# Attention, MLP and routed experts: token rows reordered in 32x32 blocks by VectorE instead of turned by TensorE

## The chip, the cores and the metric

The kernel runs on one core of a Trainium2 chip. The metric is the device time of one execution in microseconds (us), the median of three runs of the kernel before: 533.54 us (533.23 to 533.99). Two numbers stand beside it for the execution that was profiled: its time was 533.14 us, and its span, which is the stretch that the trace covers, was 531.4 us.

## The reference, cut to what matters

Three stages follow each other. All inputs are float32.

```python
# 1 attention with decay, B=2, H=8, S=768, D=64, in blocks of 64 positions -> x [1536, 512]
# 2 gated MLP, d_model 512, d_ff 1536
g = x @ w_gate
x2 = (g * sigmoid(g) * (x @ w_val)) @ w_out
# 3 top-1 experts: E=8, F=1024
logits = x2 @ router
e = argmax(logits, axis=1)
gate = softmax(logits)[e]
out[token] = gate * (relu(x2[token] @ w1[e]) @ w2[e])
```

So stage 3 needs each token's row of x2 (512 numbers) and its 8 logits, gathered by expert.

## The kernel before

There is no scheduler. Each engine has its program written out in order, and semaphores tie them together. SP (SyncE) issues nearly all loads in one queue, so an instruction on SP that waits holds back everything behind it. POOL (GpSimd) issues the gathers and scatters.

Each float32 product is made of three reduced products: a tile is split into a high part (a copy to fp32r by ScalarE, ACT) and a low part (a subtraction by VectorE, DVE), and TensorE (PE) multiplies high by high, high by low, and low by high. `split_expert` does this for one of the 8 pieces of an expert's weights, `tokens` for an expert's rows.

**MLP.** The 1536 tokens are three groups of 512. The result of a group, `x2f`, has the features on the partitions and the tokens along the free axis. An expert needs rows that can be gathered, so the tokens must come to the partitions. `rows(fin, t, where)` in the PE program turns one tile of 128 tokens with four 128x128 transposes (L974), and `rows_out` copies it from PSUM to `x2`, beside the 8 logits. `store_rows` stores 128 rows of 520 numbers to `x2_rows` in DRAM. Groups 0 and 1 are turned between other products: group 0 behind `held_out` j = 2, 4, 6, 8 and group 1 behind the hidden units f = 1 to 4 of the last group. Group 2 is turned in the tail of the MLP.

**Experts.** An expert has two tiles of 120 rows (`ROWS`), so 240 places. Tiles 0 and 1 of expert 0 have paths of their own (`gather_a`, `gather_b`, `transpose_a`, `transpose_b`). For experts 1 to 7, POOL gathers the rows into `gx[0]` and `gx[1]`, and `transpose_rows(x)` in the PE program turns them back with two times four transposes (L1163), for expert 1 ahead of the last part of expert 0, and for the others inside the expert before, after `outward(x, par, 3)`. ACT and DVE split the turned rows from PSUM into `exh` and `exl`.

In expert x the PE order is `hidden(0)`, `hidden(1)`, `outward(0)`, `hidden(2)`, `outward(1)` and so on: `hidden(f)` is 12 matmuls of 240 columns (L1174), `outward(f)` 6 matmuls of 512 (L1184). `outward(f)` waits for `ehl`, the low part of relu, which DVE makes after ACT has made `ehh`. In the same steps ACT and DVE split piece f of the next expert's weights, and at f = 5 the next expert's rows (`tokens`). SP loads the weights of an expert in four loads of 1 MB (`load_expert`), each as soon as DVE has split the piece pair that lay in that slot. In `last_expert` tile 0 goes with the hidden steps, and all of tile 1 follows (`outward_tile`, L1217).

Empty places hold an index (2048) that the gather skips.

Of the kernel before, what the change touches and what calls it, by code (L numbers as in the profile page):

```python
# [38 lines left out]
ROWS_BEHIND = (2, 4, 6, 8)  # L39
# [21 lines left out]
EMPTY = 2048  # L61
# [37 lines left out]
def bass_linear_attention_mlp_moe(nc, attn_in, lam_rows, mlp_w, router_w, expert_w, out):  # L99
    ctx = ExitStack()  # L100
    with ctx:
# [7 lines left out]
        x2_rows = nc.dram_tensor("x2_rows", [N, ROW], F32, kind="Internal").ap()  # L109
# [100 lines left out]
        x2 = sb("x2", [P, GTT, ROW], F32, region2)  # L210
# [22 lines left out]
        ys = [sb(f"ys{i}", [P, DM], F32, region2) for i in range(2)]  # L233
        region2.close()
# [73 lines left out]
        x2_stored = [sem(f"x2_stored{i}") for i in range(GTT)]  # L308
        logits_psum = sem("logits_psum")
# [23 lines left out]
        gx_landed = [sem(f"gx_landed{i}") for i in range(2)]  # L333
        exh_ready = sem("exh_ready")
# [19 lines left out]
        def expert_bufs(par):  # L354
            return ((ewh0, ewl0), (ewh1, ewl1))[par]

# [102 lines left out]
        def _(sp):  # L459
# [10 lines left out]
            for n in range(4, NT):  # L470
                sp.wait_ge(scores_ready, n - 3)
                if n >= 6:
                    sp.wait_ge(qs_ready, n - 5)
                keys_and_queries_in(n % 4, n)
                sp.wait_ge(o_ready, n - 3)
                rows_in(n % 4, n)
                if n == 6:
                    for h in range(2):
                        sp.dma_start(flat(h), mlp_w[0][:, h * GT:(h + 1) * GT]).then_inc(first_halves[h], 16)
# [69 lines left out]

            sp.wait_ge(mwl_ready, splits(1, NF1 - 1))  # L550
# [4 lines left out]
            sp.wait_ge(route, (NG - 1) * STEPS + 3)  # L555
            for t in range(GTT):
                sp.wait_ge(rows_ready, (NG - 1) * GTT + t + 1)
                sp.dma_start(x2_rows[(NG - 1) * GT + t * P:(NG - 1) * GT + (t + 1) * P, :],
                             x2[:, t, :]).then_inc(x2_stored[t], 16)
# [3 lines left out]
            n = read_passes(sp)  # L563
            with sp.Fori(2, E) as e:
                load_expert(e, e)

            def later_pass(p):
                with sp.Fori(0, E) as e:
                    load_expert(p * E + e, e)

# [6 lines left out]
        def _(pool):  # L577
# [78 lines left out]
            last_early_row = pool.to_reg((NG - 1) * GT - 1)  # L656

# [5 lines left out]

            def gather_a():
# [3 lines left out]
                for t in range(GTT):  # L668
                    pool.wait_ge(x2_stored[t], 16 * (NG - 1))
                pool.wait_ge(gx_zero, 1)  # L670
# [12 lines left out]
            def gather_b():  # L683
# [3 lines left out]
                for t in range(GTT):  # L687
                    pool.wait_ge(x2_stored[t], 16 * NG)
                pool.wait_ge(idx_ready, 1)
                fetch(gx[1], x2_rows, idx[:, E:E + 1], gx_landed[1])  # L690

            def gather(x):
                pool.wait_ge(gx_read, x * 2)
                pool.wait_ge(expo_ready, x)
                pool.wait_ge(idx_ready, 1)
                for i in range(2):
                    fetch(gx[i], x2_rows, idx[:, x + i * E:x + i * E + 1], gx_landed[i])
# [12 lines left out]
            def first_pass():  # L710
                gather_b()
                pool.wait_ge(gx_read, 1)
                fetch(gx[0], x2_rows, idx[:, 1:2], gx_landed[0])
                pool.wait_ge(expo_ready, 1)
                fetch(gx[1], x2_rows, idx[:, E + 1:E + 2], gx_landed[1])
# [8 lines left out]
            def gather_by_copy(x, base, par):  # L724
# [6 lines left out]
                for i in range(2):  # L731
                    fetch(gx[i], x2_rows, idx_now[:, 2 * par + i:2 * par + i + 1], gx_landed[i])
# [47 lines left out]
        def _(pe):  # L780
# [190 lines left out]
            def rows(fin, t, where):  # L971

                for k in range(KD):
                    last = nc.tensor.transpose(bank[:, where, k * P:(k + 1) * P], x2f[:, k, t * P:(t + 1) * P],  # L974
# [15 lines left out]
            def first_half(g, fin=None):  # L990

                for f in range(HALF):
# [3 lines left out]
                    if fin is not None:  # L996
                        if f == 0:
                            logit_product(fin)
                        if f == 1:
                            pe.wait_ge(route, fin * STEPS + 1)  # L1000
# [1223 lines left out]
```

## Time and profile before

| | |
|---|---|
| median of three runs | 533.54 us |
| the profiled execution | 533.14 us, span 531.4 us |
| PE busy | 522.7 us (98%) |
| DVE busy | 348.7 us (66%) |
| ACT busy | 253.8 us (48%) |
| POOL busy | 73.2 us (14%) |
| the chain that ended last | PE 95%, DMA 1%, issue 1% |
| mean granted TensorE clock | 0.997 of full speed |

The attention stage takes about the first 46 us of the span, the MLP runs to about 335 us, and the experts fill the rest. The chain of waits is almost all PE, so what counts is what PE executes and what makes it wait; other engines count where PE comes to wait for them.

### The profile page before, as it was taken

The numbers are of one execution on the slowest core, as the hardware profiler recorded it, in microseconds if no ns is written. First come the engines' busy times: TensorE is split into PE (matmuls) and PEld (weight loads), VectorE is DVE, ScalarE is ACT, GpSimd is POOL, SyncE is SP. The second block draws the span as 40 slices with busy tenths as digits, with TensorE's granted clock in tenths as the row PEclk, the third lists the DMA queues.
The fourth block names the chain that finished last, engine by engine and source line by source line (L and its number), as shares of the span: only waits on it lengthen the run. The fifth ranks groups of instructions, "written<-read, shape, count | busy, mean of one in ns | idle before, by whom it ended". The sixth has DMA issues, their size and how long they took to land.

```text
span 531.4 us, 8643 instructions
## 1 busy us (share of the span) xinstructions
PE 522.7 (98%) x3279; PEld 443.3 (83%) x3279; DVE 348.7 (66%) x601; ACT 253.8 (48%) x447; POOL 73.2 (14%) x86
## 2 busy tenths in 40 slices
PE   8999999999999999999999999999999999999995
PEld 7998888888888887887888888778888989888893
DVE  7889998787784737644556666567666666766620
ACT  4663564535454325543334534466555455555511
POOL 5761000000000000010000020033022130321101
PEclk9999999999999999999999999999999999999998
DMA  8995224313030305655344566267675665654001
GB/s 282 395 317 199 70 91 158 120 39 140 20 133 7 120 9 183 188 167 208 92 128 152 185 198 237 81 204 256 210 276 195 219 224 205 224 215 153 3 26 37
DMA packets 22570, 84.58 MB, mean 159 GB/s; under 512 B 3836, under 2 KB 3836, under 8 KB 18944
## 3 DMA queue, kind: packets, MB, share of 16 engines
q1 hardware_dynamic: 17664, 71.35, 38.9%
q0 software_dynamic: 3712, 10.54, 6.0%
q10 hardware_dynamic: 1152, 2.13, 1.0%
q8 instruction: 26, 0.43, 0.3%
q14 instruction: 16, 0.13, 0.1%
HBM read 75.32 MB, written 10.27 MB: 161 GB/s over the span
## 4 chain that ended last, share of the span: by engine, by line
PE 95%; DMA 1%; issue 1%; POOL 0%; SPq 0%; POOLq 0%; ACT 0%; DVE 0%
PE bank L947 18%; PE bank L872 16%; PE bank L1174 14%; PE bank L1184 13%; PE bank L880 12%; PE bank L904 6%; PE bank L1088 2%; PE bank L1107 2%; PE bank L830 2%; PE bank L792 2%; PE bank L803 2%; DMA stages<-attn_in 1%; PE bank L1163 1%; PE bank L974 1%; PE bank L1217 1%
## 5 line engine op out<-in xcount | busy, mean ns | idle before, releaser
L1639 DVE TENSOR_TENSOR ewl<-stages,ewh 128x1024 fp32r<-128x1024 f32 x50 | 60.7, 1222 | 17.2 <-ACT ewh L1261 17.2
L1261 ACT ACTIVATE ewh<-stages 128x1024 fp32r<-128x1024 f32 x50 | 52.1, 1052 | 0.3 <-DMA stages<-expert_w 0.3
L1584 ACT ACTIVATE ehh<-bank 128x240 fp32r<-128x240 f32 x48 | 17.8, 370 | 57.8 <-PE bank L1174 51.2
L644 POOL DMA_DIRECT2D stages<-expert_w x8 | 4.6, 577 | 260.4 <-DVE more_hl L1639 185.1
L1184 PE MATMUL bank<-ewh,ehl 128*120 128x512 f32 x96 | 38.0, 396 | 0.0
L1184 PE MATMUL bank<-ewl,ehh 128*120 128x512 f32 x96 | 37.8, 394 | 0.0
L1184 PE MATMUL bank<-ewh,ehh 128*120 128x512 f32 x96 | 37.8, 394 | 0.0
L659 POOL DMA_INDIRECT gx<-x_rows,idx x15 | 22.2, 1481 | 105.3 <-issue 85.1
L1174 PEld LDWEIGHTS bank<-exh,ewh 128*128 128x128 f32 x224 | 32.7, 189 | 4.2
L2132 DVE SCALAR_TENSOR_TENSOR ehl<-bank,ehh 128x240 fp32r<-128x240 f32 x48 | 19.4, 404 | 23.8 <-ACT ehh L1584 23.8
L1174 PE MATMUL bank<-exh,ewh 128*128 128x240 f32 x224 | 34.8, 278 | 0.0
L1174 PE MATMUL bank<-exh,ewl 128*128 128x240 f32 x224 | 34.5, 276 | 0.0
L872 PE MATMUL bank<-xh,gvh 128*128 128x512 f32 x128 | 34.4, 391 | 0.0
L1174 PE MATMUL bank<-exl,ewh 128*128 128x240 f32 x224 | 34.4, 276 | 0.0
L872 PE MATMUL bank<-xl,gvh 128*128 128x512 f32 x128 | 34.2, 389 | 0.0
L872 PE MATMUL bank<-xh,gvl 128*128 128x512 f32 x128 | 34.2, 389 | 0.0
L1174 PEld LDWEIGHTS bank<-exl,ewh 128*128 128x128 f32 x224 | 29.7, 191 | 0.0
L1174 PEld LDWEIGHTS bank<-exh,ewl 128*128 128x128 f32 x224 | 29.6, 190 | 0.0
L1261 ACT ACTIVATE c<-bank 128x512 f32<-128x512 f32 x30 | 17.9, 596 | 24.3 <-PE bank L947 24.3
L880 PE MATMUL bank<-hh,woh 128*128 128x512 f32 x72 | 28.7, 398 | 0.0
L872 PEld LDWEIGHTS bank<-xl,gvh 128*128 128x128 f32 x128 | 24.0, 188 | 5.0
L872 PEld LDWEIGHTS bank<-xh,gvl 128*128 128x128 f32 x128 | 24.0, 188 | 5.0
(292 smaller groups left out, 1240.6 us busy)
## 6 DMA issues: line engine op xcount, KB each, us to landing
stages<-expert_w SPq DMA_DIRECT2D x21, 1024.0 KB, 5.0
stages<-mlp_w SPq DMA_DIRECT2D x23, 768.0 KB, 4.5
stages<-attn_in SPq DMA_DIRECT2D x18, 512.0 KB, 6.9
stage<-expert_w SPq DMA_DIRECT2D x7, 1024.0 KB
stages<-expert_w POOLq DMA_DIRECT2D x8, 512.0 KB, 5.7
stages<-mlp_w SPq DMA_DIRECT2D x13, 256.0 KB, 3.0
stage<-attn_in SPq DMA_DIRECT2D x6, 512.0 KB, 6.7
held<-c SPq DMA_DIRECT2D x12, 256.0 KB, 2.0
```

The source lines that it names most:

```text
L659: nc.gpsimd.indirect_dma_start(out=dst[0:ROWS, :], out_offset=None, in_=src, in_offset=bass.IndirectOffsetOnAxis(ap=at[0:ROWS, :], axis=0) ...
L792: last = mm(bank[:, S_BANK[n % 2] + z, a * CH:(a + 1) * CH], kt[z * D:(z + 1) * D, a, :], qt[z * D:(z + 1) * D, a, :], start=True, stop=True)
L872: last = mm(bank[:, where, :], wt[:, k, :], (xh, xl)[x][:, k, g * GT:(g + 1) * GT], start=(at == 0), stop=(at == 3 * KD - 1))
L880: last = mm(bank[:, d, :], (woh, wol)[w][wo][:, d * P:(d + 1) * P], (hh, hl)[x][h][:, :], start=(f == 0 and n == 0), stop=True, skip_group ...
L904: last = mm(bank[:, d, :], (woh, wol)[w][j % 3 + 1][:, d * P:(d + 1) * P], (hh, hl)[x][j % 3 + 1][:, :], start=(j == 0 and n == 0), stop=True,
L947: last = mm(where, mix(i, w)[:, n * KH * P + k * P:n * KH * P + (k + 1) * P], moving[i][x][:, k, :], start=(first and at == 0), stop=(at = ...
L1174: last = mm(bank[:, H_BANK + f % 2, 0:CAP], expert_bufs(par)[w][:, f, k * P:(k + 1) * P], (exh, exl)[z][par][:, k, 0:CAP], start=(at == 0) ...
L1184: last = mm(bank[0:ROWS, Y_BANK + t, 0:DM], (ehh, ehl)[z][f % 2][:, t * ROWS:(t + 1) * ROWS], expert_bufs(par)[w][:, f, KD * P:], start=(f ...
L1261: return nc.scalar.activation(dst, src, ACT.Copy)
L1584: nc.scalar.activation(ehh[f % 2][:, :], bank[:, H_BANK + f % 2, 0:CAP], ACT.Relu).then_inc(ehh_ready, 1)
L1639: V.tensor_tensor(dst, src, high.bitcast(F32), ALU.subtract).then_inc(inc, 1)
L2132: V.scalar_tensor_tensor(out=ehl[f % 2][:, :], in0=bank[:, H_BANK + f % 2, 0:CAP], scalar=0.0, in1=ehh[f % 2][:, :].bitcast(F32), op0=ALU.max,
```

## The change

Two kinds of turning leave PE.

1. **Groups 0 and 1 of the MLP.** DVE turns a tile with one instruction, a stream transpose, which transposes each 32x32 block of a 128x512 tile on its own and moves no block to other partitions. So a row of `x2` on partition (b, i), with b the block of 32 partitions, holds for each of 16 blocks of 32 tokens a piece of 128 numbers. The blocks are brought to their rows by the store: one store for each b, of 512 pieces of 512 bytes (`store_blocks`). The features of a row lie in another order (`block_order`: k inside, four by four). Group 2 is still turned by PE, and ACT's copy puts it in that order. The logits have a tile (`x2_logits`) and a store of their own, of 32-byte pieces.
2. **Rows of experts 1 to 7.** POOL gathers into `gy`. SP stores both tiles to a DRAM buffer `xg`, waits for that store, and loads `gt` with four loads of 32 partitions, 256 pieces of 512 bytes each, and the logits (`lg`) with a fifth. DVE then makes the turned tiles with one stream transpose each, from `gt` to the same two PSUM banks. SP does the store and the loads of expert e right behind the four weight loads of e.

Also: the tiles `exh` and `exl` are read in two strips of 120 columns with a pitch of 128; ACT and DVE split 128 columns per tile instead of 120; empty places hold the index 1536, a spare row that is gathered like any other; in `last_expert` the first product of tile 1 stands ahead of the wait for the last `ehl`; and the two loads of the first MLP weights (`sig`, `hid`) are issued at attention tile 11 instead of 6, and read by ACT after tile 8 instead of 7.

```diff
 # SP
-                if n == 6:
+                if n == NT - 1:
                     for h in range(2):
                         sp.dma_start(flat(h), mlp_w[0][:, h * GT:(h + 1) * GT]).then_inc(first_halves[h], 16)
...
+            def store_rows(x):
+                for i in range(2):
+                    sp.wait_ge(gy_landed[i], x * 16)
+                    sp.dma_start(xg[i * P:i * P + ROWS, :], gy[i][0:ROWS, :]).then_inc(xg_stored, 16)
+
+            def load_rows(x):
+                sp.wait_ge(xg_stored, x * 32)
+                for b in range(NB):
+                    sp.dma_start(gt[b * BLOCK:(b + 1) * BLOCK, :, :],
+                                 xg[:, b * P:(b + 1) * P].rearrange("(q i) c -> i q c", i=BLOCK)
+                                 ).then_inc(gt_landed, 16)
+                sp.dma_start(lg[:, :, :], xg[:, DM:].rearrange("(t r) e -> r t e", r=P)).then_inc(lg_landed, 16)
...
+            store_rows(1)
+            load_rows(1)
             with sp.Fori(2, E) as e:
                 load_expert(e, e)
+                turn_rows(e)
 # POOL
             def gather(x):
-                pool.wait_ge(gx_read, x * 2)
-                pool.wait_ge(expo_ready, x)
+                if x >= 2:
+                    pool.wait_ge(gt_landed, (x - 1) * (16 * NB))
+                    pool.wait_ge(lg_landed, (x - 1) * 16)
 # PE
-                        if 1 <= f <= GTT:
-                            pe.wait_ge(rows_ready, fin * GTT + f - 1)
-                            rows(fin, f - 1, ROWS_BANK)
...
-                    if f == 4 and more:
-                        transpose_rows(x + 1)
...
-                transpose_rows(1, True)
...
+                outward_tile(x, 0, 1)
                 pe.wait_ge(ehl_ready, x * NF2 + NF2)
                 outward_tile(x, NF2 - 1, 0)
-                for f in range(NF2):
+                for f in range(1, NF2):
                     outward_tile(x, f, 1)
 # ACT
+            def store_blocks(fin, b):
+                act.wait_ge(rows_ready, fin * GTT + GTT)
+                act.dma_start(x2_rows[fin * GT:(fin + 1) * GT, b * P:(b + 1) * P].rearrange("(q i) c -> i q c", i=BLOCK),
+                              x2[b * BLOCK:(b + 1) * BLOCK, :].rearrange("i (q c) -> i q c", c=P)
+                              ).then_inc(x2_stored[b], 16)
 # DVE
+            def turn_rows(fin, t):
...
+                V.transpose(x2[:, t * DM:(t + 1) * DM].rearrange("p (a j k) -> p a k j", a=NB, k=KD),
+                            x2f[:, :, t * P:(t + 1) * P].rearrange("p k (a i) -> p a k i", a=NB)).then_inc(rows_ready, 1)
...
+            def turn_tokens(x, i):
+                dve.wait_ge(gt_landed, x * (16 * NB))
+                dve.wait_ge(exh_ready, x * 2)
+                V.transpose(bank[:, T_BANK + i, :].rearrange("p (k q i) -> p q k i", k=KD, q=NB),
+                            gt[:, i * NB:(i + 1) * NB, :].rearrange("p q (j k) -> p q k j", k=KD)).then_inc(gx_read, 1)
...
                         split_expert(1 - par, x + 1, f, f // 2)
+                        if f in (3, 4):
+                            turn_tokens(x + 1, f - 3)
```

On SP, between the last load of expert 1's weights and the loop over the weights of experts 2 to 7, before:

```order
L562 DMA stage<-expert_w 128x2048 [waits gx_landed1,slots_ready]
L449 TENSOR_LOAD passes [waits slots_ready]
L449 ISA x2
L564 UNCONDITIONAL_BRANCH
L564 ISA
L548 ISA [waits ewl_ready]
L548 DMA stages<-expert_w 128x2048
```

and in the changed program:

```order
L605 DMA stage<-expert_w 128x2048 [waits gx_landed1,slots_ready]
L471 TENSOR_LOAD passes [waits slots_ready]
L471 ISA x2
L579 DMA xg<-gy 120x520 [waits gy_landed0,eh_psum,spares_set]
L579 DMA xg<-gy 120x520 [waits gy_landed1]
L584 DMA gt<-xg 32x8x128 [waits xg_stored]
L584 DMA gt<-xg 32x8x128 x3
L587 DMA lg<-xg 128x2x8
L611 UNCONDITIONAL_BRANCH
L611 ISA
L570 ISA [waits ewl_ready]
L570 DMA stages<-expert_w 128x2048
```

The loads of expert 2's weights now stand behind the store and the five loads of expert 1's rows. The same seven transfers close each turn of the loop.

On DVE, in an expert, steps f = 3 to 5 (`ehl` is the low part of the hidden tile, `ewl` that of the next expert's weights, `exl` that of its rows). These are rows of the first expert that runs in this form; before:

```order
L2132 SCALAR_TENSOR_TENSOR ehl<-bank,ehh 128x240 [waits ehh_ready]
L1639 TENSOR_TENSOR ewl<-stages,ewh 128x1024 [waits ewh_ready]
L1639 TENSOR_TENSOR exl<-bank,exh 128x4x120 [waits exh_ready] x2
```

and in the changed program, from f = 3 on:

```order
L2187 SCALAR_TENSOR_TENSOR ehl<-bank,ehh 128x240 [waits ehh_ready]
L1676 TENSOR_TENSOR ewl<-stages,ewh 128x1024 [waits ewh_ready]
L2166 STREAM_TRANSPOSE bank<-gt 128x4x4x32 [waits exh_ready,gt_landed]
L2187 SCALAR_TENSOR_TENSOR ehl<-bank,ehh 128x240 [waits ehh_ready]
L1676 TENSOR_TENSOR ewl<-stages,ewh 128x1024 [waits ewh_ready]
L2166 STREAM_TRANSPOSE bank<-gt 128x4x4x32 [waits exh_ready,gt_landed]
L2187 SCALAR_TENSOR_TENSOR ehl<-bank,ehh 128x240 [waits ehh_ready]
L1676 TENSOR_TENSOR ewl<-stages,ewh 128x1024 [waits ewh_ready]
L1676 TENSOR_TENSOR exl<-bank,exh 128x4x128 [waits exh_ready] x2
```

Two transposes came in, the first behind the weight piece of step 3 and ahead of the `ehl` of step 4, and both wait for the loads.

## Rows read from the trace of the kernel before

**Rows 1.** Busy time of the engines in two stretches; the columns stand in the first line.
```profile
core 0: us, PE busy (x) PEld busy (x) DVE busy (x) ACT busy (x) POOL busy (x), PEclk, DMA share, GB/s
200.00:300.00 100.00, 100.00 (x482) 80.44 (x481) 59.33 (x122) 42.01 (x68) 2.98 (x5) 1.00 0.50 163
400.00:500.00 100.00, 100.00 (x671) 89.37 (x670) 66.04 (x99) 54.35 (x94) 20.37 (x16) 1.00 0.55 189
```

**Rows 2.** Chain of waits, the transposes: start us, us, what.
```profile
211.56 0.44 PE bank L974 x4
...
362.44 0.82 PE bank L1163 x8
```

**Rows 3.** Chain of waits, products of experts 1 and 2.
```profile
366.06 2.72 PE bank L1174 x24
...
388.87 2.71 PE bank L1174 x24
...
397.08 1.39 PE bank L1184 x6
```

**Rows 4.** Chain of waits, a moving operand in one strip and in four.
```profile
238.21 5.44 PE bank L872 x24
...
341.17 1.87 PE bank L1088 x8
```

**Rows 5.** Timeline of DVE from 361 to 370: start us, us, line, op, names, shapes.
```profile
361.15 0.69 DVE L2075 TENSOR_TENSOR turned<-bank,turned 128x512 fp32r<-128x512 f32 x1 [1.09 <-ACT turned L1261]
363.50 1.22 DVE L1639 TENSOR_TENSOR exl<-bank,exh 128x480 fp32r<-128x480 f32 x2 [1.66 <-ACT exh L1261]
...
365.12 2.35 DVE L1639 TENSOR_TENSOR ewl<-stage,ewh 128x1024 fp32r<-128x1024 f32 x2
...
368.04 0.40 DVE L2132 SCALAR_TENSOR_TENSOR ehl<-bank,ehh 128x240 fp32r<-128x240 f32 x1
```

**Rows 6.** Timeline of ACT, the split of expert 1's rows.
```profile
362.89 1.03 ACT L1261 ACTIVATE exh<-bank 128x480 fp32r<-128x480 f32 x2 [1.27 <-PE bank L1163]
```

**Rows 7.** Timeline of DVE, steps 3 and 4 of expert 2.
```profile
398.46 1.22 DVE L1639 TENSOR_TENSOR ewl<-stages,ewh 128x1024 fp32r<-128x1024 f32 x1 [0.54 <-ACT ewh L1261]
400.27 0.41 DVE L2132 SCALAR_TENSOR_TENSOR ehl<-bank,ehh 128x240 fp32r<-128x240 f32 x1 [0.59 <-ACT ehh L1584]
```

**Rows 8.** Timeline of SP: last weight loads of expert 1 and of expert 3.
```profile
350.34 0.33 SPq L562 DMA_DIRECT2D stage<-expert_w  x1
...
388.86 0.33 SPq L548 DMA_DIRECT2D stage<-expert_w  x1
```

**Rows 9.** Timeline of POOL, gathers for expert 0 and for expert 1.
```profile
346.20 1.72 POOL L659 DMA_INDIRECT gx<-x_rows,idx  x1 [15.69 <-DVE idx L2099]
348.22 1.11 POOL L659 DMA_INDIRECT gx<-x_rows,idx  x1 [0.30 <-issue]
```

**Rows 10.** DMA issues: names, queue, count, KB each, median us to landing.
```profile
stages<-expert_w SPq DMA_DIRECT2D x21, 1024.0 KB, 5.0
...
x_rows<-x ACTq DMA_DIRECT2D x8, 260.0 KB, 5.6
x_rows<-x SPq DMA_DIRECT2D x4, 260.0 KB, 2.3
```

**Rows 11.** Timeline of SP, the stores of group 2.
```profile
340.01 2.14 SPq L558 DMA_DIRECT2D x_rows<-x  x4
```

**Rows 12.** DMA queues from 340 to 344: queue, packets, MB, share of 16 engines.
```profile
q1 hardware_dynamic: 576, 1.07, 70.1%
```

**Rows 13.** Timeline of DVE, first reader of sig's split.
```profile
45.10 0.68 DVE L1639 TENSOR_TENSOR gvl<-sig,gvh 128x512 fp32r<-128x512 f32 x1
```

**Rows 14.** Timeline of the end: last wait of PE and last copy.
```profile
518.16 0.40 PE L1217 MATMUL bank<-ewl,ewh 128*120 128x512 f32 x1
...
518.76 0.49 PE L1217 MATMUL bank<-ewh 128*120 128x512 f32 x1 [0.20 <-DVE ewl L2148]
...
525.27 0.69 ACT L1608 ACTIVATE ys<-bank,gate_now 120x512 f32<-120x512 f32 x1 [4.82 <-PE bank L1217]
```

More of the change, by code:

```diff
@@ L333, in bass_linear_attention_mlp_moe @@
         gx_landed = [sem(f"gx_landed{i}") for i in range(2)]
+        gy_landed = [sem(f"gy_landed{i}") for i in range(2)]
+        xg_stored = sem("xg_stored")
+        spares_set = sem("spares_set")
+        gt_landed = sem("gt_landed")
+        lg_landed = sem("lg_landed")
         exh_ready = sem("exh_ready")
@@ L969, in turn_logits, with rows @@
                 last.then_inc(logits_psum, 1)
-            def rows(fin, t, where):
+            def rows(t):
                 for k in range(KD):
-                    last = nc.tensor.transpose(bank[:, where, k * P:(k + 1) * P], x2f[:, k, t * P:(t + 1) * P],
+                    last = nc.tensor.transpose(bank[:, t, k * P:(k + 1) * P], x2f[:, k, t * P:(t + 1) * P],
                                                ident[:, :])
@@ L1154, in _ @@
             half_outward(0, 1, 6, 12)
-            def transpose_rows(x, first=False):
-                for i in range(2):
-                    pe.wait_ge(gx_landed[i], (x + 1) * 16)
-                    pe.wait_ge(exl_ready, x * 2)
-                    if first and i:
-                        pe.wait_ge(y0_ready, 1)
-                    for k in range(KD):
-                        last = nc.tensor.transpose(bank[:, T_BANK + i, k * P:k * P + ROWS],
-                                                   gx[i][0:ROWS, k * P:(k + 1) * P], ident[0:ROWS, 0:ROWS])
-                    last.then_inc(gx_read, 1)
             def hidden(x, par, f):
@@ L1188, in outward, with expert @@
                         last.then_inc(y_psum, 1)
-            def expert(x, par, more):
+            def expert(x, par):
                 pe.wait_ge(exl_ready, x * 2 + 2)
@@ L1247, in _ @@
             first_expert()
[L1248 removed]
+            expert(1, 1)
             n = read_passes(pe)
@@ L1931, in choose @@
             def choose(fin):
-                now = x2[:, :, DM:]
+                now = x2_logits[:, :, :]
                 dve.wait_ge(logits_psum, fin + 1)
-                for t in range(GTT if fin else 0):
-                    dve.wait_ge(x2_stored[t], fin * 16)
+                if fin:
+                    dve.wait_ge(logits_stored, fin * 16)
                 step(fin, 1, V.tensor_reduce(
@@ L2154, in experts @@
                     split_expert(0, base, f, f // 2)
+                for i in range(2):
+                    turn_tokens(base, i)
                 tokens(base, 0)
```

155 lines of the change are left out of this document (93 added, 62 removed).

## The prediction, written before the changed kernel ran

> **What bounds the kernel now.** I read the busy times first, then the chain of waits, then the timelines of the engines that PE could come to wait for. PE is busy for all of 100 us in the MLP and for all of 100 us in the experts, at the full clock, and the chain that ended last is PE from one end to the other [rows 1]. So an instruction that leaves PE shortens the kernel by its place in the chain, as long as nothing else then comes too late. DVE has 41 us free in the first of these stretches and 34 us in the second [rows 1]. The question is not whether DVE has the time, but whether the turned rows reach it in time.
>
> **What leaves PE.** Groups 0 and 1 of the MLP lose eight groups of four transposes. In the chain such a group is worth 0.44 us [rows 2]: 3.52 us. Experts 1 to 7 lose eight transposes each, 0.82 us in each of the seven places, of which one is shown [rows 2]: 5.74 us.
>
> In the last expert three matmuls move in front of the last wait. The matmul after the wait starts 0.60 us after the one before it, where the step is 0.23 us (24 matmuls in 5.44 us) [rows 4, 14]. So 0.37 us of waiting are filled. ACT's last copy starts when PE's last matmul ends [rows 14], so it moves up by as much. Tile 0 is ready about 0.3 us later, and nobody waits for it. Gain: 0.37 us.
>
> **What the MLP pays.** DVE makes eight transposes of 128x512. No row shows one. Its other operations on 128x512 take 0.69 us [rows 5]; I take that. Then 5.5 us are added over some 90 us in which DVE is idle two fifths of the time. A unit of the last group is 36 matmuls long on PE, 8.2 us at 0.23 [rows 4], in which DVE by its share is idle for 3.3, and it gets at most two transposes, 1.4: nothing on the chain. The stores become 512 pieces of 512 bytes each, but the first reader of the rows is the gather for expert 0, in the second half of the last group. The move of sig and hid costs nothing as well: they are issued when the scores of tile 7 are done, four of twelve tiles before the end of a stage of 46 us, some 15 us ahead of it. A load of 1 MB takes 5.0 us [rows 10], and DVE reads their split at 45.10 [rows 13].
>
> **What the matmuls of the experts pay.** Their moving operand now lies in two strips of 120 columns. The trace has such a case: the moving operand of L1088 is four strips of 128, and eight take 1.87 us, 0.23 each, as the 24 of L872 with one strip [rows 4]. So I take 0. That ACT and DVE split 512 columns instead of 480 adds 0.03 us to an operation that is not waited for.
>
> **The first expert.** DVE is free at 361.84, when its subtraction is done [rows 5]. It used to wait 1.66 us for ACT [rows 5]; now two transposes of 0.69 fill that time, to 363.2. ACT needs 0.5 us for the second copy [rows 6] and DVE 0.6 for its low part: 364.4, against 364.72 before. PE, without its 0.82 us, comes to expert 1 at 365.24 instead of 366.06 [rows 3], so this is in time. But the first `ehl`, behind two splits (2.35 us) and more, was ready at 368.44 [rows 5], and would be some 0.3 us sooner, while PE now asks for it at 365.24 + 2.72 = 367.96. PE waits about 0.35 us. Of the 0.82 us here 0.47 are left (they are in the 5.74 above: take off 0.35).
>
> Are the rows there at 361.84? POOL's gather was issued by 347.92, and SP's load that waits for it went out at 350.34: 2.4 us [rows 8, 9]. The gathers of expert 1 follow at 348.2 and 349.6 (the second waits for nothing new) and land by about 353.1. The two stores stand in SP's queue behind a load of 1 MB issued at 350.34, which takes 5.0 us [rows 8, 10], to 355.3. Four stores of 260 KB were issued from 340.01 in 2.14 us, the last 0.35 before that ends, and land 2.3 us after issue [rows 10, 11], so all four are done in 4.1 us, and two more in the queue are worth about 1.4 us: 356.7. Then four loads of 0.33 us to issue and 2.3 to land: 3.6, with 0.3 for the wait, 360.6. That leaves 1.2 us.
>
> **Experts 2 to 7.** Let S be the start of an expert on PE (388.87 for expert 2 [rows 3]). SP issues the last weight load at S [rows 8], and the stores of the next expert's rows right behind. The load is done at S + 5.0, the stores at S + 6.4, the loads of `gt` at S + 10.3. DVE would start the first transpose when the piece of step 3 is split, at 399.68, that is S + 10.8 [rows 7]. Just in time. And it may be later: PE's `outward(4)` needs the `ehl` of step 4. It comes after `outward(2)` begins (397.08 [rows 3]) plus 5.5 us, at 402.6; less 0.69 for the transpose and 0.41 for the `ehl` [rows 5, 7] this gives 401.5, S + 12.6. So there are 2.3 us of slack, and the gain of 0.82 is kept whole. In the steps 3 and 4 DVE works 1.63 us and then 2.3 of 2.74 us. The weights of the expert after next are issued some 3 us later than before, and are needed 13 us after that. In the change's own order `gather(x)` waits for `gt` of x - 1, which is there more than 10 us before SP needs the rows.
>
> How late can the loads be? No row shows pieces of 512 bytes. From below, they are limited by issue and landing: 3.6 us, as above. From above, a piece costs as much as one of 2080 bytes: the four stores of 260 KB are 512 such pieces, and kept 70.1% of the engines busy for 4 us, 2.8 us [rows 12], so 1024 pieces take 5.6, with 2.3 to land 7.9 us, and end at S + 14.6. I take the lower end, since the bytes are half of those of the four stores.
>
> By the Trainium skill (DMA: Bandwidth & Descriptors, Specifications) 512 bytes is the smallest transfer at full rate. By that rule the lower end holds, as in the sum; no row before shows it. The same skill (VectorE: DVE Perf Modes, The three transpose paths) gives 311 ns for a VectorE transpose of 128x128 in bf16. Four times that is an estimate of 1.24 us for 128x512, against the 0.69 of the rows; by it the first expert would cost 1.1 us more, and the time would be 525.4.
>
> **The sum.** 3.52 + 5.74 + 0.37 - 0.35 = 9.28 us. The profiled execution took 533.14 us, of which 1.74 lie around the span; less 9.28 this is 523.9. The median is 0.40 above the profiled execution: 524.3 us.
>
> **Rivals.**
> - *Rows a little late.* The stores' landing is worse under load: ACT's stores of the same size took 5.6 us where SP's took 2.3 [rows 10]. If the store takes 3.3 us longer, `gt` comes at S + 13.6, 1.0 us after the limit, six times, and 2.1 us after 361.84 in the first expert: 8.1 of the 9.3 us are given back: 532.4. If it takes half of that longer, only the first expert loses 0.5: 524.8. For it: at S the scatters of the last expert run on the same engines. Against it: SP's own stores had a quiet queue, and so has this one once the weight load is through. Between the two lie times of 525 to 532.
> - *Transposes dear.* If one takes 2.4 us (two operations on 128x1024 took 2.35), DVE ends step 4's transpose and the `ehl` of step 5 about 1.1 us too late, six times, and the first expert loses 3.4: near 534, no change. At 1.8 us or less the six lose nothing.
> - *Small pieces, the other side.* If each piece of 512 bytes costs what one of 2080 costs, `gt` comes at S + 14.6, 2.0 us late in each of six experts, and 3.1 us late in the first. PE waits 15.1 us for 9.3 us gained: 539.4, slower. It decides from 1.33 us late in each of the seven on. For it: no trace here has such pieces. Against it: they carry a quarter of the bytes.
> - *It doesn't do what it says* would need transposes of these experts still on PE; the order shows none.
>
> **How the numbers follow.** The forecast 0.68, with its own range of 523 to 526.5; rows a little late, between 526.5 and 532.4, 0.14; dear transposes at 0.06, of which half end near no change; small pieces 0.10; 0.02 is left for what I did not see. A measurement of this kernel can tell about 0.2% (1.07 us) from no change. Faster: 0.68 + 0.14 + 0.03 = 0.85; same 0.04; slower 0.11. The range reaches from 522.8 to 531.5.
>
> **What would show it.** The span near 522; no L974 between 200 and 285 us; PE busy without a gap from 200 us to the last expert but for 0.3 to 0.5 us at the first `ehl` of expert 1; an expert on PE lasting 21.98 instead of 22.80 us; the stream transpose at 0.69 us; DVE's wait ahead of the first one of an expert ended by a DMA for less than 1.8 us. If PE waits for `ehl` in step 4 of every expert, and DVE before it for `gt`, the forecast is wrong in the chain store to load. If DVE is busy at that time, it is wrong in the price of the transpose. If an expert's matmuls are dearer than 1.35 us per twelve, the strips are the reason.

## The result, and the profile after

The changed kernel takes 543.06 us (541.04 to 545.82, 5 runs) against 533.54 us (533.20 to 533.99, 5 runs): a ratio of 1.018 (95% interval 1.0150 to 1.0211). The forecast was 524.3 us, with a range that reached to 531.5 us for the late rows; the result lies outside it, on the other side of no change. The profiled execution took 545.82 us with a span of 543.8 us, against 531.4 us for the span before. It is the slowest of the five, 2.8 us above their median.

The table of what each engine waited for begins with PE in the changed kernel (us in total, times, longest); before, none of the first two lines was there.

```profile
PE bank L1220 <- DVE ehl L2187: 10.7, 6, 4.1
PE bank L1209 <- DVE exl L1676: 2.7, 1, 2.7
...
PE bank L1143 <- ACT sig L1568: 0.6, 1, 0.6
```

The same table for DVE says what DVE was late with: blocks of `gt`, in all seven experts.

```profile
DVE bank L2166 <- DMA gt<-xg: 21.9, 7, 5.6
```

Stretches of the changed kernel, with the same columns as [rows 1]: PE stands in 360 to 370, in 380 to 390 and again and again behind 400, where it was busy throughout before. The granted clock (PEclk) is 0.83 in the stretch from 360 and 0.66 in that from 380, so part of these ran at the lower of the two levels, 1.2 GHz; before, it was 1.00 there.

```profile
360.00:370.00 10.00, 7.30 (x37) 6.42 (x36) 7.39 (x12) 4.51 (x7) 3.96 (x4) 0.83 0.98 326
...
380.00:390.00 10.00, 5.89 (x27) 5.05 (x26) 6.14 (x9) 2.61 (x5) 2.21 (x2) 0.66 0.86 290
...
400.00:450.00 50.00, 45.70 (x288) 40.39 (x287) 32.94 (x48) 24.51 (x41) 8.70 (x8) 0.97 0.74 241
450.00:500.00 50.00, 48.07 (x312) 42.27 (x311) 35.63 (x53) 26.74 (x43) 8.75 (x8) 1.00 0.81 269
```

The chain of waits (start us, us, what) no longer is PE from end to end. For the rows of experts 3 to 7 it goes from DVE's last split over SP's last weight load (419.20) and the stores behind it to the loads of `gt`, over one transpose to one `ehl`, and only then back to PE. This is the worst of these five; PE waits 3.3 us.

```profile
417.81 1.24 DVE ewl L1676
...
419.20 0.33 SPq L570
...
420.07 10.16 DMA xg<-gy
...
430.25 0.32 SPq L584
...
432.02 2.74 DMA gt<-xg
...
435.87 0.40 DVE ehl L2187
...
436.31 1.75 PE bank L1220 x6
438.06 2.55 PE bank L1209 x12
```

Read it with the last two rows: after the wait PE makes the twelve products of L1209 in 2.55 us; they take 1.35 us at full clock. Part of the wait is paid for a second time.

The longest wait for `ehl`, 4.1 us, is that of the rows of expert 2, and its chain is another one: the gather is issued only when the blocks of expert 1's rows have landed, and it takes 9.04 us itself. SP had issued the last weight load at 368.46 and stood until 373.55.

```profile
364.49 9.04 DMA gy<-x_rows,idx
373.55 6.02 DMA xg<-gy
...
380.93 2.91 DMA gt<-xg
...
384.86 0.40 DVE ehl L2187
...
385.30 2.91 PE bank L1220 x6
```

**The account.** There are 14.0 us of waits, of which 0.6 belong to the MLP's term below. Read by single microseconds, the granted clock is at half from 366.0 to 369.4, from 383.1 to 389.9 and from 437.7 to 441.1 us. Half of that time is lost, but 2.2 us of the second stretch lie inside the wait itself, where PE has nothing to lose. That leaves 1.7, 2.3 and 1.7 us: 5.7 us. The first product of the MLP came 0.5 us later in this execution than in the one before. After a wait the next six products take 1.65 us in the chain instead of 1.39, for example here, where the clock is at 1.00:

```profile
410.65 1.65 PE bank L1220 x6
...
413.67 1.40 PE bank L1220 x6
```

Five such restarts are 1.3 us. The terms of the gain, as measured below, are 8.9 us. 531.4 - 8.9 + 13.4 + 5.7 + 0.5 + 1.3 = 543.4 us, and the span is 543.8.

### The profile page after: what moved, and what is told of

It is laid out like the page before. It is cut to its first block and busy times, and to the rows that moved or that the text cites. A ratio compares the mean times of both kernels' runs of the same rounds, so it can differ in the third digit from the quotient of the medians.

```text
span 543.8 us, 8532 instructions
## 1 busy us (share of the span) xinstructions
PE 521.5 (96%) x3191; PEld 441.0 (81%) x3191; DVE 368.7 (68%) x623; ACT 252.4 (46%) x432; POOL 69.0 (13%) x86
## 5 line engine op out<-in xcount | busy, mean ns | idle before, releaser
L1220 PE MATMUL bank<-ewh,ehh 128*120 128x512 f32 x96 | 39.5, 412 | 10.7 <-DVE ehl L2187 10.7
L1209 PEld LDWEIGHTS bank<-exh,ewh 128*128 128x128 f32 x224 | 34.5, 196 | 7.8 <-DVE exl L1676 3.1
L1209 PE MATMUL bank<-exh,ewh 128*128 128x240 f32 x224 | 35.9, 284 | 2.7 <-DVE exl L1676 2.7
L1209 PE MATMUL bank<-exl,ewh 128*128 128x240 f32 x224 | 36.1, 285 | 0.0
L1209 PE MATMUL bank<-exh,ewl 128*128 128x240 f32 x224 | 35.5, 282 | 0.0
L1209 PEld LDWEIGHTS bank<-exl,ewh 128*128 128x128 f32 x224 | 31.3, 199 | 0.0
L1209 PEld LDWEIGHTS bank<-exh,ewl 128*128 128x128 f32 x224 | 30.8, 196 | 0.0
L1220 PEld LDWEIGHTS bank<-ewh,ehh 128*120 128x120 f32 x96 | 17.8, 185 | 15.5 <-DVE ehl L2187 12.8
L2166 DVE STREAM_TRANSPOSE bank<-gt 128x512 f32<-128x512 f32 x14 | 15.1, 1086 | 21.9 <-DMA gt<-xg 21.9
```

The lines of the kernel that those rows point to most:

```text
L1209: last = mm(bank[:, H_BANK + f % 2, 0:CAP].rearrange("p (t r) -> p t r", r=ROWS), expert_bufs(par)[w][:, f, k * P:(k + 1) * P], (exh, exl) ...
L1220: last = mm(bank[0:ROWS, Y_BANK + t, 0:DM], (ehh, ehl)[z][f % 2][:, t * ROWS:(t + 1) * ROWS], expert_bufs(par)[w][:, f, KD * P:], start=(f ...
L2166: V.transpose(bank[:, T_BANK + i, :].rearrange("p (k q i) -> p q k i", k=KD, q=NB), gt[:, i * NB:(i + 1) * NB, :].rearrange("p q (j k) -> ...
```

## The experiments

All were timed against the kernel before. Two theories stood after the result. QUEUE: the rows come late because the stores stand in the wrong place of SP's DMA queue, behind the last weight load. PRICE: something in the new work is dearer than taken, small pieces, transposes or strips.

### e1: the MLP's part and the end alone

For the experts the code of before was kept (the gathered tiles turned by TensorE); the rest is the change.

```
+ TURNED_BEHIND = (3, 4, 6, 9)
-                         if 1 <= f <= GTT:
-                             rows(fin, f - 1, ROWS_BANK)
+                 outward_tile(x, 0, 1)
                  pe.wait_ge(ehl_ready, x * NF2 + NF2)
...
```

> The MLP part of the change alone: groups 0 and 1 are turned by VectorE and stored in blocks, the first product of tile 1 in the last expert stands ahead of the wait; the rows of experts 1 to 7 are gathered and turned by TensorE as before. If this part is as sized, 8 groups of transposes at 0.44 us and the 0.37 us at the end leave: 533.5 - 3.9 = 529.6 us, and the granted clock stays at 1. If the VectorE transposes (now measured at 1.09 us) or the stores in 512-byte pieces make TensorE wait, it stands between 530.5 and 534.

Measured: 530.65 us (530.18 to 530.70), ratio 0.9939 (0.9926 to 0.9953): by the ratio 3.3 us of the 3.9, at the edge of the second range of the expectation. The MLP's part is a gain, somewhat less than its size. The trace shows two places where it went, and neither is one that the expectation named. First, ACT's copies now write with a stride of four words (`block_order`), and PE waits 0.6 us for `sig` behind them; this is ACT's timeline.

```profile
334.96 3.86 ACT L1276 ACTIVATE x<-bank 128x512 f32<-128x512 f32 x4 [4.03 <-PE bank L1000]
```

Four copies take 3.86 us; before, three took 1.58 and the fourth 0.60 us. Second, the chain has the eight transposes of the gathered tiles at 0.95 us, where [rows 2] have 0.82: they read the same block order, in the other direction. That is 0.13 us in each of seven places, 0.9 us, which this kernel pays and the whole change does not.

```profile
375.06 0.95 PE bank L1177 x8
385.64 2.72 PE bank L1188 x24
```

### e2: the stores ahead of the last weight load

```
-            with sp.Fori(2, E) as e:
-                load_expert(e, e)
-                turn_rows(e)
+            for e in range(2, E):
+                for q in range(PIECES):
+                    sp.wait_ge(ewl_ready, (e - 1) * NF2 + (2 * q + 2))
+                    if q == 3:
+                        turn_rows(e)
+                    sp.dma_start(stage[q][:, :], expert_w[e, q]).then_inc(landed[q], 16)
```

> The changed kernel with one order altered on SP: for experts 2 to 7 the store and the loads of the rows are issued ahead of the last weight load instead of behind it, after the same wait (the loop over the experts is written out). Theory QUEUE (the store is slow because it stands behind 1 MB of weights in SP's queue): the stores land within 3 to 4 us of issue instead of 8 to 10, gt is there about 8.5 us after an expert starts, TensorE no longer waits for ehl in step 4; only the late rows of expert 1 remain: 527 to 531 us. Theory PIECES (the way over DRAM in small pieces is slow by itself, whatever stands ahead): the chain stays at 12 us and more and the time at 540 to 546. Theory TRANSPOSE (VectorE at 2 x 1.09 us per expert is what is late): no change of the time either, and VectorE does not wait for gt.

Measured: 529.35 us (529.26 to 530.99), ratio 0.9926 (0.9909 to 0.9943), as theory QUEUE said. One place in one queue is worth 13.7 us. The transposes, the pieces of 512 bytes and the strips are all still there, so none of them made the changed kernel slower than before. Of its waits for `ehl` 2.8 us are left, and none after 381 us; the wait for `exl` is 1.8 us. The DMA issues of e2, with the columns of [rows 10], show the stores at 3.3 us.

```profile
xg<-gy SPq DMA_DIRECT2D x12, 243.8 KB, 3.3
```

### e3: the stores and loads behind the third weight piece

The loop of e2, with `turn_rows(e)` behind the load of piece 2 and with `sp.wait_ge(expo_ready, e)` ahead of it.

> As the kernel with the store first, but the rows go one weight load earlier still, between the third and the fourth (with a wait for ScalarE's exp of the expert before). QUEUE: nothing is left to wait for in either, so the same time within 1 us, 527 to 531; a store here stands behind the third weight load, so it lands late again (7 to 9 us) without anyone waiting. If the scatters, which run at an expert's start, were what slowed the store, this one lands in 3 to 4 us and the one before does not. PIECES: also fast here, since the chain has 6 us more room; then the store in the kernel before must be slow.

Measured: 528.96 us (528.81 to 530.51), ratio 0.9908 (0.9893 to 0.9924). No wait for `ehl` is left. What is left is one wait of 2.9 us for `exl` at the start of expert 1, and in the profiled execution the clock behind it, 0.72 in 360 to 370 and 0.94 in 370 to 380: 3.1 us more, without the part that lies in the wait. That execution took 530.51 us at a mean clock of 0.990; the other three took 528.81 to 529.05 us at 0.997 to 0.999, so they did not pay this, and the median does not hold it. The stores landed in 5.0 us (median of 14), although they stand behind the third weight load: the expectation said 7 to 9, or 3 to 4, and missed this.

### e8: the same moment, another queue

The kernel is the changed one; only the engine that issues the stores of experts 2 to 7 differs.

```
 # SP
-                turn_rows(e)
+                load_rows(e)
 # ACT, behind its last operation of expert x
+            def store_rows(x):
+                act.wait_ge(ewl_ready, x * NF2)
+                for i in range(2):
+                    act.wait_ge(gy_landed[i], x * 16)
+                    nc.scalar.dma_start(xg[i * P:i * P + ROWS, :], gy[i][0:ROWS, :]).then_inc(xg_stored, 16)
```

> The changed kernel (543.06 us) with one difference: for experts 2 to 7 the two stores of a gathered tile (xg from gy) are issued by ACT on ACT's DMA queue, at the moment at which SP issued them (when the last weight piece of the expert before is issued); SP still issues the loads of the blocks, behind the same wait. Nothing is earlier; only the queue differs. Theory QUEUE (the stores stood behind the 1 MB weight piece because one queue passes its packets in turn): the stores are through within 4 us of their issue instead of 7.4 to 10.2, PE's waits for ehl fall from 10.7 us to under 3, the time is 529 to 532. Rival ENGINES (the 16 DMA engines are full of weights, and packets wait there whatever queue they come from): 7 to 10 us from issue to landing again, and 541 to 545 us.

Measured: 538.32 us (536.29 to 543.87), ratio 1.0102 (1.0044 to 1.0159). As a time it fits neither theory, and the trace shows that the edit has a fault of its own: an engine that waits for a gather holds its other work behind it. ACT stood 6.70 us until 372 for the gather of expert 2. Until 399 it did nothing else for 4.33 us, 2.52 of them to issue the stores beside a full queue.

```profile
369.72 2.42 ACTq L1613 DMA_DIRECT2D xg<-gy  x2
372.18 0.37 ACT L1628 ACTIVATE ehh<-bank 128x240 fp32r<-128x240 f32 x1 [6.70 <-DMA gy<-x_rows,idx]
```

Behind these two places ACT holds nothing up for long, and the two kernels can be compared. PE's waits from 405 to 525 us, first in the changed kernel, then in this one:

```profile
PE bank L1220 <- DVE ehl L2187: 6.6, 5, 3.3
```

```profile
PE bank L1220 <- DVE ehl L2196: 0.3, 1, 0.3
```

The DMA issues of e8 (columns as in [rows 10]):

```profile
xg<-gy ACTq DMA_DIRECT2D x12, 243.8 KB, 5.7
```

In the chain of the changed kernel they took 7.38 to 10.16 us (five of them), behind a weight load of 1 MB in the same queue; here 5.7, beside that load in another queue; in e2 3.3, ahead of it. So both theories hold a part: a part of the delay is the place in the queue, and a part stays when the queue is another one. That this second part comes of the weights on the same engines is the likely reading; e12 tests it for the gathers alone.

### e7: expert 1's rows ahead of its last weights, too

```
+            store_rows(1)
+            load_rows(1)
             sp.dma_start(stage[3][:, :], expert_w[1, 3]).then_inc(landed[3], 16)
-            store_rows(1)
-            load_rows(1)
...
                 split_second_expert(5)
+                turn_tokens(1, 0)
                 low_half(1, 1)
-                turn_tokens(1, 0)
```

> Rows early for experts 2 to 7, and for expert 1 the last weight load goes behind the rows' store and loads, and VectorE makes the first transpose in the 1.1 us in which it waits ahead of the last subtraction. QUEUE: the gather for expert 1 also landed late (8.3 us) behind that megabyte; TensorE's wait of 2.7 us at the start of expert 1 goes, 0.3 to 1 us at the first ehl stays: 524 to 526.5 us. If the late first expert has another cause, 527 to 530 as the two before.

Measured: 530.92 us (530.13 to 531.31), ratio 0.9941 (0.9926 to 0.9956): a miss, 2 us slower than e3, which it was to mend. The wait for `exl` is gone, since the gather landed in 4.3 us instead of 8.3. But the wait came back one expert later. The chain:

```profile
358.91 1.09 POOL gy L719
...
360.30 10.48 DMA gy<-x_rows,idx
...
370.80 4.52 DMA xg<-gy
...
376.68 2.96 DMA gt<-xg
...
380.66 0.39 DVE ehl L2191
```

The gather for expert 2 takes 10.48 us: at 356.12 to 358.36 SP had issued four weight pieces of 1 MB at once. The DMA share (last column but one) of the stretch behind it:

```profile
360.00:370.00 10.00, 9.27 (x59) 8.07 (x58) 8.60 (x14) 5.72 (x9) 4.17 (x3) 1.00 1.02 359
```

### e9: expert 2's rows ahead of three of its weight pieces

```
-                if x >= 2: pool.wait_ge(gt_landed, (x - 1) * (16 * NB)) ...
+                if x >= 2: pool.wait_ge(xg_stored, (x - 1) * 32)
...
             def store_rows(x):
+                if isinstance(x, int) and x > 1:
+                    sp.wait_ge(gt_landed, (x - 1) * (16 * NB))
+                    sp.wait_ge(lg_landed, (x - 1) * 16)
...
-                    if q == 2:
+                    if q == (0 if e == 2 else 2):
+                        store_rows(e)
                         sp.wait_ge(expo_ready, e)
-                        turn_rows(e)
+                        load_rows(e)
```

> The kernel e7 (530.92 us) with the rows of expert 2 earlier: the gather of expert x waits only until the rows of x-1 are stored, not until their blocks are loaded (6 us sooner for expert 2), and the stores and loads of expert 2 stand behind the first weight piece of expert 2 instead of behind the third. Theory: the 3.7 us wait for ehl at 381 us and the 3.4 us at half clock behind it go (3.7 + 1.7 = 5.4), and what is left is the sum of the prediction with no late rows: 524 to 526.5 us. Rival: three weight pieces of expert 2 are now behind the rows and come late in turn, or the gather still takes 8 to 10 us beside the weights: a wait of 2 to 5 us stays and the time is 528 to 531.

Measured: 536.45 us (535.61 to 537.12), ratio 1.0055 (1.0041 to 1.0068): the cause that the rival named, and more than 5 us above its range. Now the rows are there (DVE waits for `gt` 1.6 us, once), and the weights are late, since SP stands at the wait for the gather with three weight loads behind it. The chain:

```profile
355.16 8.44 DMA stage<-expert_w
...
370.48 9.39 DMA stages<-expert_w
...
380.98 1.23 DVE ewl L1683
382.21 0.33 DVE ehl L2194
...
382.58 2.91 PE bank L1227 x6
```

### e12: less weight beside the rows

The kernel is e7, and the first three pieces of expert 2 cut to half (the other half of each buffer keeps the piece before, so its output for expert 2 is wrong; it only serves to ask about time).

```
+                    some = EW if e == 2 and q < 3 else 2 * EW
-                    sp.dma_start(stage[q][:, :], expert_w[e, q]).then_inc(landed[q], 16)
+                    sp.dma_start(stage[q][:, 0:some], expert_w[e, q][:, 0:some]).then_inc(landed[q], 16)
```

> The kernel e7 (530.92 us) with half of each of the first three weight pieces of expert 2 left out (512 KB instead of 1 MB each; the other half of the buffer keeps the piece before, so the output for expert 2 is not the reference's; ACT and VectorE work on as much as before). Theory BANDWIDTH (the gather of expert 2 took 10.5 us from 360.3 because the 16 DMA engines are full of the weights issued at 356 to 358, share 1.02 in 360:370): with 1.5 MB less of them the gather lands 4 us or more sooner, the wait for ehl of 3.7 us at 381 goes, and the time is 525 to 527.5. Rival SLOW GATHER (it takes 8 to 10 us by itself, or the chain behind it is the whole of it): the gather still lands after 369, the wait stays at 3 us or more, and the time 530 to 531.

Measured: 526.17 us (525.98 to 526.82), ratio 0.9868 (0.9851 to 0.9884), so 1.5 MB less of weights are worth 3.9 us by the two ratios. That is in the range of theory BANDWIDTH. The gather of expert 2 takes 7.82 us where it took 10.48 (4 less were expected), the clock stays at 1.00 from 340 to 500 us, and of the 4.4 us of waits for `ehl` 1.4 are left, none above 1.0. So volume beside the rows costs time in the first experts. It is not the whole of the slow gather: 7.82 us are still well above the 4.3 us that the gather of expert 1 takes in e7 and here.

### e11: TensorE for expert 1, VectorE for the other six

The edit is made on e3; nothing of expert 1 is stored or loaded.

```
-            store_rows(1)
-            load_rows(1)
 # PE, first_expert
                 half_outward(1, 0, 3, 12)
+                for i in range(2):
+                    pe.wait_ge(gy_landed[i], 16)
...
+                    for k in range(KD):
+                        last = nc.tensor.transpose(bank[:, T_BANK + i, k * P:k * P + ROWS],
+                                                   block_order(gy[i][0:ROWS, 0:DM])[:, k], ident[0:ROWS, 0:ROWS])
                 half_outward(1, 1, 0, 12)
```

> The kernel e3 (528.96 us) with the rows of expert 1 turned by TensorE again, eight transposes of the gathered tiles between the second experts' matmuls as in the kernel before (2 x 0.82 us for the two tiles of an expert are 0.82 in sum by the rows of before); the rows of experts 2 to 7 by VectorE as in e3. Nothing of expert 1 is stored or loaded any more. Theory FIRST EXPERTS (what e2, e3, e7 and e9 lack of the predicted gain is lost in 350 to 390 us alone, where the rows of experts 1 and 2 and 4 MB of weights come at once): the 2.9 us wait for exl at 365 us and the 3.4 us of half clock behind it go and 0.82 us of TensorE come back: e1's 530.65 - 6 x 0.82 = 525.7, 524.5 to 526.7 us. Rival SPREAD (the removed transposes are worth less than 0.82 us each group, because matmuls slow down beside the fuller DMA queues and VectorE): e1 to e3 differ by 1.7 us, so 528 to 529 us even without the wait.

Measured: 527.29 us (526.50 to 527.51), ratio 0.9880 (0.9863 to 0.9896): the best complete kernel here, 1.2% faster than before, and between the two ranges. (An expert's eight transposes are 0.82 us together [rows 2]; the "2 x 0.82" of the expectation is a slip.) The rival is refuted by the chain, in which the first products of experts 3 to 7 follow each other in 21.98 us, against 22.94 in e1. Against e3 the gain is 1.5 us by the ratios, and the two intervals just overlap. Counted from the first product of the MLP, which this profiled execution reached 1.4 us later than that of e1, it takes 4.1 us less than e1. The transposes of six experts, at the 0.95 us that they take in e1, are 5.7 us; less the wait below and the slow restart behind it that is 4.5. The table of PE's waits has only this behind the MLP, and the clock is 1.00 from 350 to 500:

```profile
PE bank L1225 <- DVE ehl L2206: 0.9, 1, 0.9
```

### e10: each transpose twice

On e9, a second stream transpose into the same bank behind each, with a semaphore between the two.

```
+                for done in (turned_once, gx_read):
+                    V.transpose(...).then_inc(done, 1)
+                    if done is turned_once:
+                        dve.wait_ge(turned_once, x * 2 + i - 1)
```

> e9 with each stream transpose of a rows' tile made twice (the second behind the first), 14 more of 1.09 us on DVE, at f = 3 and 4 of each expert. Theory DVE TIGHT: between two ehl of those strips (2.74 us) DVE works 0.40 + 1.22 + 1.09 already, so a second transpose delays ehl by up to 1.1 us, less the lead of under one strip: 1 to 2 us per expert of PE waiting, 7 to 14 us over e9. Rival COVERED: DVE is idle 20% of the stretch and takes it in its gaps: under 1 us over e9.

Measured: 541.30 us (538.83 to 543.51), ratio 1.0143 (1.0110 to 1.0176), 4.85 us over e9. Both expectations missed, the truth lies between. The chain gives the price of an expert: the first products of experts follow each other in 23.12 us where 21.98 stood, 1.14 more for 2.2 us of extra transposes. So about half of the added work is covered, and the other half reaches PE, as a wait of 0.46 us for `ehl` with its restart and as smaller delays around it.

```profile
418.63 2.72 PE bank L1217 x24
441.75 2.72 PE bank L1217 x24
```

### e6: the end alone

```
+                outward_tile(x, 0, 1)
                 pe.wait_ge(ehl_ready, x * NF2 + NF2)
                 outward_tile(x, NF2 - 1, 0)
-                for f in range(NF2):
+                for f in range(1, NF2):
```

> The kernel before with the order at the end of the last expert alone changed (the six matmuls of chunk 0 of the second tile ahead of the wait for the last ehl). Theory: they fill the wait of 0.20 us and the matmuls behind it start without a stall, 0.37 us in all: ratio 0.9993. Rival: the wait moves to y_psum's readers at the end and nothing is gained: ratio 1.0000. Either lies near what can be told apart; over 0.2% in either direction would speak against both.

Measured: 533.25 us (532.67 to 534.70, 11 runs) against 533.68; ratio 0.9996 (0.9987 to 1.0005). That agrees with 0.37 us and with nothing at all; it can't be told apart.

## Why the prediction was wrong

**The step that failed** is the chain from store to load: "The load is done at S + 5.0, the stores at S + 6.4, the loads of `gt` at S + 10.3", with a limit of S + 12.6. In the changed kernel S is still the moment of the last weight load. The longest pieces of the chain for the rows of experts 3 and 5 to 7 (those of expert 4's rows, 10.16 and 2.74 us, stand above):

```profile
397.61 7.38 DMA xg<-gy
406.35 2.75 DMA gt<-xg
...
447.30 8.12 DMA xg<-gy
456.79 3.00 DMA gt<-xg
470.75 7.86 DMA xg<-gy
479.97 2.90 DMA gt<-xg
493.84 7.55 DMA xg<-gy
502.88 2.76 DMA gt<-xg
```

With the weight loads at 395.95, 419.20, 446.43, 469.88 and 492.97 the stores are done at S + 9.0, 11.0, 9.0, 8.7 and 8.4, and the blocks are there at S + 13.2, 15.6, 13.4, 13.0 and 12.7. Against S + 12.6 that is 4.7 us late in the five together, and with the dearer transpose, which moves the limit to S + 12.2, 6.7; PE waited 6.6 us in this stretch. In e8 the four loads go out at S + 7.4 to 7.7, which puts the blocks at S + 11.9 to 12.2 (12.9 once, where the four took 2.7 us to issue), and PE waits 0.3, once. So the limit was right and the arrival wrong by 2.4 to 5.3 us, against a slack of 2.3. Two things are in it. The stores: they "are worth about 1.4 us" behind the load, from four stores in a quiet queue [rows 10 to 12]; the load itself now lands in 6.1 to 8.4 us in these five instead of 5.0, and the stores end 2.0 to 4.6 us later than said. Their neighbour in the rows was in sight: ACT's stores of the same size took 5.6 us [rows 10]. The loads: 3.9 us were taken from the stores' end to the blocks, 4.1 to 4.5 are seen, since each of the later three takes 0.45 us to issue.

**Expert 2.** A second step failed here: "In the change's own order `gather(x)` waits for `gt` of x - 1, which is there more than 10 us before SP needs the rows." The blocks of expert 1 were there at 362.13 and SP wanted the rows of expert 2 at 368.8, 6.7 us later; the gather took until 373.55. The wait of 4.1 us behind it is the longest of the kernel.

**What sits behind it: the DMA engines as a shared resource.** The prediction read their share only in a stretch of 4 us [rows 12]. The column was there: 0.55 in 400 to 500 [rows 1]. In the changed kernel it is 0.77 there, in 360 to 370 it is 0.98. Rows that are stored and loaded again cost 1 MB more per expert, and many landings near them take longer: in these kernels gathers took up to 10.5 us and weights up to 9.4. A landing time of before is no constant. The link from share to landing time was tested once, in e12; for the stores behind the weight load it is argued.

**The first expert.** Forecast: gather landed by 353.1, blocks at 360.6, needed at 361.84. These are times of the trace before, and the MLP's gain moves all of them. In the changed kernel DVE's subtraction ends at 359.53 instead of 361.84, 2.3 us sooner, so in its frame the forecast says 350.8, 358.3 and 359.5. Seen: the second gather was issued at 347.30 and took 8.28 us, to 355.6; blocks at 362.1, 2.6 us after DVE could have used them; PE's wait 2.7 us. The gather ran beside a weight load issued at 348.17; in e7, with that load behind the rows, it took 4.26 us.

**The clock.** No term of the prediction had it. Three of the waits (2.7, 4.1 and 3.3 us) were followed by products at 1.2 GHz, 5.7 us lost in all, beside 13.4 us of waits. In the profiled execution of e3 one wait of 2.9 us cost 3.1 more. The other runs of e3 show that such a price is not paid each time.

**The terms of the gain were nearly right.**
- Experts: 5.74 forecast. The expert on PE lasts 21.98 instead of 22.80 us, as said; the chain of e9:

```profile
418.19 2.73 PE bank L1216 x24
440.17 2.73 PE bank L1216 x24
```

- MLP: 3.52 forecast, 2.8 measured. In e1 expert 1 starts at 362.71 us instead of 366.06 [rows 3], 3.35 sooner, but its first product of the MLP was already 0.67 sooner (the first input lands differently in each execution: with the same attention program it was at 45.75 in e1 and at 47.44 in e10), which leaves 2.68, and 0.13 more for the dearer transposes. What lacks is the wait for `sig` of 0.6 us; the copies of `x` with a stride had no line in the sum. The chains of e1 and then of before:

```profile
45.75 14.32 PE bank L898 x62
...
362.71 2.69 PE bank L1188 x24
```

```profile
46.42 13.60 PE bank L872 x59
```

- End: 0.37, not refuted.
- Strips: 0 was right. In e11 the products of an expert take 275 to 277 ns, as before (276 to 278); in the changed kernel 282 to 285, by the slow clock.
- DVE: 0.69 us was taken for a stream transpose; it takes 1.09 (1.05 to 1.11). The rival "transposes dear" said that up to 1.8 us nothing is lost in experts 2 to 7 and that at 2.4 us about 1.1 us are. The doubling, 2.2 us in a step, costs PE 1.14 per expert, so it had the place right and the price a little low. By the Trainium skill (VectorE: DVE Perf Modes, The three transpose paths) the estimate was 1.24 us; it was nearer than the row of another operation, and the measurement decides.

**The rivals.** "Rows a little late" named the mechanism that came true, at 0.14, and ended it at 532.4 by two bounds: 3.3 us for a late store and no price for the clock. Against it stood that "SP's own stores had a quiet queue, and so has this one once the weight load is through"; with its own queue quiet, the engines still were not. "Small pieces, the other side" gave 15.1 us of waiting, near the measured 13.4, with the wrong cause: that is luck. The loads with pieces of 512 bytes land 2.7 us after issue by the profile, and e2 and e3 have just as many and are faster than before. With this agrees the Trainium skill (DMA: Bandwidth & Descriptors, Specifications), which calls 512 bytes the smallest transfer at full rate. The block stores of the MLP leave it open: they landed in 8.4 us where the stores of whole rows took 5.6 (medians of eight on ACT's queue), but they are also issued in another rhythm, and PE never waited for them.

**Where the rest of the gain of e2, e3 and e7 went:** to 350 to 390 us, where gathers for two experts and five weight pieces meet. Every order of them tried there left something late (`exl` 2.9, `ehl` 3.7, weights 5.9), and only less volume, half weights or one expert less to store, brought the waits behind the MLP down to 1.4 and 0.9 us.

## What to carry to other kernels

A round trip through memory that is put behind a big load in the same queue waits for the load and then for its own turn; price it with the landings of the busiest stretch, not of a quiet one, and put it ahead of the load wherever the load has more slack. Where a change moves one stage forward, the times of the next have to be read in the moved frame. Where a chain of landings has a slack of 2 us, a forecast without a loss needs the DMA share of that stretch as a term, and a price for the clock behind a wait. An engine or queue that waits for a gather holds all that is behind it, so each move of such a wait has to be followed to what now stands behind.

## What the runs showed of the hardware

- A VectorE stream transpose of 128x512 in fp32, written to PSUM with a stride, took 1.09 us (1.05 to 1.11).
- Stores of 244 KB landed in 3.3 us ahead of a weight load of 1 MB, in 5.7 us beside it on another queue, in 7.4 to 10.2 us behind it on the same queue (medians, and the range of five). In e3, behind the third weight load, the median was 5.0 us, so the place alone does not set it.
- Gathers of 120 rows of 2080 bytes took from 4.1 to 10.5 us: 10.48 us with four loads of 1 MB, 7.82 with three of them halved.
- ACT's copy of 128x512 from PSUM took about 1 us with a stride of four words in its output and 0.60 without.
- TensorE's transposes of a tile in block order: 0.95 us for eight against 0.82.
- Six TensorE products behind a wait took 1.65 us in the chain, 1.39 without one, at the same clock of 1.00.
- TensorE's granted clock fell to its lower level, 1.2 GHz, around three of its waits in the changed kernel (2.7, 4.1 and 3.3 us): 0.66 on average in 380 to 390. It also fell behind a wait of 2.61 us in e8. It stayed at 1.00 around waits of 1.8 and 2.0 us in e2, of 2.37 us in e9 and of 2.67 us in e10. So the length of the wait alone does not say whether it falls.
